# kv in 13 pieces by thirds of its rows, tile 0 scored third by third, and constant products between the pieces

## What is computed

```python
B, N, C = q.shape                      # 1, 12288, 128
kv_pool = kv.reshape(B, H // 4, 4, W // 4, 4, C).mean(axis=(2, 4))   # H = 384, W = 32
k = v = kv_pool.reshape(B, -1, C) @ w_sr                             # 768 keys
s = scale * (q @ k.transpose(0, 2, 1))
a = np.exp(s - s.max(-1, keepdims=True))
a /= a.sum(-1, keepdims=True) + 1e-09
x = a @ v
h = x @ w_in1;  x = (h / (1 + exp(-1.702 * h))) @ w_out1             # d_ff = 2048
h = x @ w_in2;  out = (h * clip(h + 3, 0, 6) / 6) @ w_out2
```

## Time and profile before

| | us |
|---|---|
| median of 3 runs (1280.7 to 1281.02) | 1280.78 |
| the profiled execution | 1280.32 |
| its span in the profile | 1278.6 |
| TensorE busy in the span | 1270.0 |
| VectorE, ScalarE busy | 1034.1, 1027.4 |

### The profile page before, as it was taken

The page is one execution under the profiler, slowest core; times in us unless marked ns, Lnnn a source line. Parts: engine busy times, 40 slices in busy tenths (PEclk is TensorE's granted clock), DMA queues, the critical chain, the costliest instruction groups (busy, mean ns, idle before and its releaser), DMA issues.

```text
span 1278.6 us, 18310 instructions
## 1 busy us (share of the span) xinstructions
PE 1270.0 (99%) x5800; PEld 1055.4 (83%) x5800; DVE 1034.1 (81%) x1084; ACT 1027.4 (80%) x1216; POOL 34.4 (3%) x46
## 2 busy tenths in 40 slices
PE   8999999999999999999999999999999999999998
PEld 7888888888888888888888888888888888888887
DVE  5788887888878878888788888887888878887768
ACT  3888877888788888887788878888888778887776
POOL 1800000000000000000000000000000000000000
PEclk9999999999999999999999999999999999999999
DMA  8421321303213123032130220311303213022001
GB/s 280 126 44 40 75 46 28 74 9 65 57 17 74 30 44 74 0 74 49 25 74 13 60 63 11 74 34 40 74 0 74 49 25 74 18 47 67 1 9 17
DMA packets 183685, 65.69 MB, mean 51 GB/s; under 512 B 104560, under 2 KB 176368, under 8 KB 183408
## 3 DMA queue, kind: packets, MB, share of 16 engines
q1 hardware_dynamic: 182576, 65.30, 22.3%
q10 hardware_dynamic: 1088, 0.13, 0.1%
HBM read 22.87 MB, written 6.34 MB: 23 GB/s over the span
## 4 chain that ended last, share of the span: by engine, by line
PE 97%; SPq 1%; DMA 1%; DVE 0%; ACT 0%; issue 0%; DVEq 0%
PE pair L1082 14%; PE pair L1083 14%; PE pair L1086 14%; PE bank_av L1082 9%; PE bank_av L1083 9%; PE bank_av L1086 9%; PE bank_out L1086 7%; PE bank_out L1083 7%; PE bank_out L1082 7%; PE score_banks L1086 2%; PE score_banks L1083 2%; PE score_banks L1082 2%; DMA kv_sb<-in_kv_dram 1%; SPq L354 0%; SPq L362 0%; SPq L366 0%
## 5 line engine op out<-in xcount | busy, mean ns | idle before, releaser
L912 DVE TENSOR_TENSOR mid_lo<-work,mid_hi 128x1024 fp32r<-128x1024 f32 (+1 forms) x193 | 233.9, 1212 | 112.5 <-ACT mid_hi L628 112.4
L1082 PE MATMUL pair<-x_hi,w_hi 128*128 128x512 f32 (+1 forms) x774 | 300.7, 388 | 0.0
L1083 PE MATMUL pair<-x_hi,w_lo 128*128 128x512 f32 (+1 forms) x774 | 300.0, 388 | 0.0
L1086 PE MATMUL pair<-x_lo,w_hi 128*128 128x512 f32 (+1 forms) x774 | 299.9, 387 | 0.0
L589 ACT ACTIVATE work<-pair 128x1024 f32<-128x1024 f32 x184 | 189.2, 1028 | 120.8 <-PE pair L1086 118.5
L904 DVE SCALAR_TENSOR_TENSOR work<-work,pair 128x1024 f32<-128x1024 f32 (+1 forms) x194 | 232.9, 1201 | 15.3 <-ACT work L616 14.6
L891 DVE TENSOR_TENSOR mid_lo<-work,mid_hi 128x1024 fp32r<-128x1024 f32 x184 | 223.6, 1215 | 25.1 <-ACT mid_hi L604 25.0
L616 ACT ACTIVATE work<-pair,half 128x1024 f32<-128x1024 f32 (+1 forms) x194 | 213.1, 1099 | 4.3 <-PE pair L1086 4.2
L628 ACT ACTIVATE mid_hi<-work 128x1024 fp32r<-128x1024 f32 (+1 forms) x193 | 201.8, 1046 | 2.3 <-DVE work L904 2.3
L604 ACT ACTIVATE mid_hi<-work 128x1024 fp32r<-128x1024 f32 x184 | 194.7, 1058 | 1.6
L1082 PEld LDWEIGHTS pair<-x_hi,w_hi 128*128 128x128 f32 x774 | 145.3, 188 | 33.7 <-ACT work L589 4.2
(11 more groups left out here) (175 smaller groups left out, 1560.2 us busy)
## 6 DMA issues: line engine op xcount, KB each, us to landing
p_keys<-p_turned SPq DMA_DIRECT2D x368, 96.0 KB, 2.2
inv_b<-inv_dram SPq DMA_DIRECT2D x23, 256.0 KB, 3.2
out_dram<-y_sb SPq DMA_DIRECT2D x92, 64.0 KB, 2.4
q_raw<-in_q_dram SPq DMA_DIRECT2D x88, 64.0 KB, 2.0
kv_sb<-in_kv_dram SPq DMA_DIRECT2D x6, 768.0 KB, 9.4
w_raw<-in_moe_w_in_dram SPq DMA_DIRECT2D x2, 1024.0 KB, 8.0
kv_sb<-in_kv_dram SPq DMA_DIRECT2D x6, 256.0 KB, 8.1
inv_dram<-inv_t SPq DMA_DIRECT2D x92, 0.5 KB
```

The lines of the kernel that those rows point to most:

```text
L912: dve.tensor_tensor(in_pair(mid_lo[mid2(t, p)], t, p, c), in_pair(act2[p % 2], t, p, c), in_pair(mid_hi[mid2(t, p)], t, p, c), ALU.subtrac ...
L1082: pe.matmul(dst, a_hi, b_hi, start=start, stop=False)
L1083: pe.matmul(dst, a_lo, b_hi, start=False, stop=False)
L1086: return pe.matmul(dst, a_hi, b_lo, start=False, stop=stop)
```

## The change

kv is loaded in 13 pieces by thirds of its rows: 128 image rows at a time, one row for each partition, two column groups (4 KB for each partition, 512 KB) in a piece, and the last two pieces one group (256 KB). Tile 0's q goes behind the fourth piece with a row of 2 KB for each partition, tile 1's q behind the last piece without a wait. A third of the rows gives a third of the keys (256), so the parts are now 256, 256, 128 and 128 keys, and a pooling product has 32 moving columns. VectorE adds four pixels to two for pieces 0 to 5 and to one for the others. One constant product of 288 columns stands between the early pieces.

Tile 0 is scored by thirds: all four slots against the first third of the keys between pieces 4 and 5, the second third around pieces 10 to 12, the last third behind the last piece. `early_maximum` takes the maximum of a slot over 512 keys, `late_maximum` that of two slots over the last 256, and a minimum (the values are negated) joins them for two slots at once. The high part of slot 0's turned probabilities is made by VectorE in place of ScalarE. GpSimd splits the inverse behind its first weight piece. PSUM banks are handed out anew. `PARTS` is 4, `SLOTS` 4 and `WIDE` 512. Cut to its core:

```diff
+        PART_AT = [0, CHUNK_KEYS, 2 * CHUNK_KEYS, 2 * CHUNK_KEYS + 128, KEYS]
+        PART_POOL = [bank_av[:, 0:CHUNK_KEYS], bank_av[:, 0:CHUNK_KEYS], bank_av[:, 0:128], bank_av[:, 128:256]]
+        PART_KEYS = [bank_out[:, 0:CHUNK_KEYS], bank_out[:, 0:CHUNK_KEYS], bank_out[:, 0:128], bank_out[:, 128:256]]
+        PARTS = 4
+
+        PIECES = [(a, g, 2) for a in range(CHUNKS) for g in range(0, KV_GROUPS, 2)][:-1] + [(2, 6, 1), (2, 7, 1)]
+        PART_PIECES = [4, 8, 10, 13]
+        SUMMED_FROM = 6
...
+        SECOND_BANK, FIFTH_BANK = pair[0][:, 512:1024], pair[1][:, 0:512]
+        VALUES_IN = [SECOND_BANK[:, 0:CHUNK_KEYS], FIFTH_BANK[:, 0:CHUNK_KEYS], SECOND_BANK[:, 0:128],
+                     bank_av[:, 256:384]]
...
+            def load_kv(a, first, groups, loaded):
+                src = kv_chunks[a][:, first * R * C:(first + groups) * R * C]
+                at = (a * KV_GROUPS + first) * R * C
+                sp.dma_start(kv_sb[:, at:at + groups * R * C], src).then_inc(loaded, 16)
+
+            for n, (a, first, groups) in enumerate(PIECES):
+                load_kv(a, first, groups, kv_loaded[n])
+                if n == 0:
+                    sp.dma_start(w_sr_sb[:, :], w_sr).then_inc(w_sr_loaded, 16)
+                if n == 3:
+                    sp.dma_start(q_raw[:, :], q_first).then_inc(q0_loaded, 16)
+            for n in range(4):
+                sp.dma_start(q_raw1[32 * n:32 * (n + 1), :], q_second[n]).then_inc(q1_loaded, 16)
...
-                if piece == 2:
+                if piece == 1:
...
+            q_high_first()
             pooled_copy(0)
             k_hi_copy(0)
-            q_high_first()
             v_hi_copy(0)
             pooled_copy(1)
+            k_hi_copy(1)
+            v_hi_copy(1)
             pooled_copy(2)
-            k_hi_copy(1)
             k_hi_copy(2)
-            v_hi_copy(1)
+            v_hi_copy(2)
+            pooled_copy(3)
+            k_hi_copy(3)
+            v_hi_copy(3)
             q1_copy()
             exponential(0, 0)
             exponential(0, 1)
-            p_hi_first(0)
             exponential(0, 2)
             p_hi_first(1)
             exponential(0, 3)
...
+            def add_pixels(n):
+                a, first, count = PIECES[n]
+                at = (a * KV_GROUPS + first) * R * C
+                groups = kv_sb[:, at:at + count * R * C].rearrange("p (g n) -> p g n", g=count)
+                dve.wait_ge(kv_loaded[n], 16)
+                half = dve.tensor_tensor(groups[:, :, 0:2 * C], groups[:, :, 0:2 * C], groups[:, :, 2 * C:4 * C],
+                                         ALU.add)
+                if n < SUMMED_FROM:
+                    half.then_inc(kv_added, 1)
+                    return
+                half.then_inc(kv_half_added, 1)
+                dve.wait_ge(kv_half_added, n - SUMMED_FROM + 1)
+                dve.tensor_tensor(groups[:, :, 0:C], groups[:, :, 0:C], groups[:, :, C:2 * C],
                                   ALU.add).then_inc(kv_added, 1)
 
...
+            def early_maximum(s):
+
+                if s < 2:
+                    dve.wait_ge(early_scored, 1)
+                else:
+                    dve.wait_ge(scores_ready, SLOTS)
+                at = first_scores_at(s, 0)
+                dve.reduce_max(early_max[:, s:s + 1], score_banks[:, at:at + WIDE], AX_X,
+                               negate=True).then_inc(max_part_ready, 1)
+
+            def late_maximum(m):
+                dve.wait_ge(scores_ready, 2 * m + 2)
+                at = first_scores_at(2 * m, CHUNKS - 1)
+                late = score_banks[:, at:at + 2 * CHUNK_KEYS].rearrange("p (s n) -> p s n", s=2)
+                dve.reduce_max(late_max[:, 2 * m:2 * m + 2], late, AX_X, negate=True).then_inc(max_part_ready, 1)
+                dve.wait_ge(max_part_ready, 3 * m + 3)
+                dve.tensor_tensor(neg_max[:, 2 * m:2 * m + 2], early_max[:, 2 * m:2 * m + 2],
+                                  late_max[:, 2 * m:2 * m + 2], ALU.min).then_inc(max_ready, 2)
+
+            def p_hi_first():
+                dve.wait_ge(pt_ready, 1)
+                dve.tensor_scalar(first_in_chunks(p_high, 0), turned_in(0), 1.0, None,
+                                  ALU.mult).then_inc(pt_hi_first_ready, 1)
...
+            for n in range(5):
+                add_pixels(n)
+            q_low_first()
             k_lo_part(0)
-            add_row_pixels(KV_GROUPS - 2, 0)
-            add_row_pixels(KV_GROUPS - 2, 1)
-            q_low_first()
-            add_row_pixels(KV_GROUPS - 2, 2)
-            add_row_pixels(KV_GROUPS - 1, 0)
-            add_row_pixels(KV_GROUPS - 1, 1)
-            add_row_pixels(KV_GROUPS - 1, 2)
+            add_pixels(5)
             v_lo_part(0)
+            for n in range(6, 10):
+                add_pixels(n)
             k_lo_part(1)
+            for n in range(10, 13):
+                add_pixels(n)
             k_lo_part(2)
-            maximum(0, 0)
+            v_lo_part(2)
             v_lo_part(1)
-            maximum(0, 1)
-            maximum(0, 2)
+            early_maximum(0)
+            k_lo_part(3)
+            early_maximum(1)
+            late_maximum(0)
+            v_lo_part(3)
+            early_maximum(2)
+            early_maximum(3)
+            late_maximum(1)
+            p_hi_first()
             p_lo_first(0)
-            maximum(0, 3)
             p_lo_first(1)
+            inverse_first()
...
+            def pool_piece(n):
+
+                a, first, count = PIECES[n]
+                part = [n < end for end in PART_PIECES].index(True)
+                if part > 0 and n == PART_PIECES[part - 1]:
+                    pe.wait_ge(pooled_ready, part)
+                pe.wait_ge(kv_added, n + 1)
+                pixels = 2 if n < SUMMED_FROM else 1
+                for g in range(first, first + count):
+                    at = (g - 4 if part == PARTS - 1 else g) * GROUP_KEYS
+                    for w in range(pixels):
+                        col = ((a * KV_GROUPS + g) * R + w) * C
+                        last = pe.matmul(PART_POOL[part][:, at:at + GROUP_KEYS], kv_sb[:, col:col + C],
+                                         patch[:, 0, :], start=w == 0, stop=w == pixels - 1)
+                if n + 1 in PART_PIECES:
...
+            def keep_busy(times, into=pair[2]):
 
                 for _ in range(times):
-                    pe.matmul(pair[2][:, 0:rows * GROUP_KEYS], ident[:, :],
-                              patch[:, 0:rows, :].rearrange("p a n -> p (a n)"), start=True, stop=True)
...
-            for g in range(1, 4):
-                pool_group(g)
-                keep_busy(3 if g < 3 else 1, rows=2)
+            keep_busy(3)
+            pool_piece(0)
+            keep_busy(1)
+            pool_piece(1)
+            keep_busy(1)
+            pool_piece(2)
+            keep_busy(1)
+            pool_piece(3)
+            turn_q_first(0)
             pe.wait_ge(w_sr_loaded, 16)
             keys_of(0)
-            pool_group(4)
             values_of(0)
-            turn_q_first(0)
-            pool_group(5)
-
-            pool_loaded_row(6, 0)
-            pool_loaded_row(6, 1)
+            keep_busy(1)
+            pool_piece(4)
             pe.wait_ge(k_lo_ready, 1)
             pe.wait_ge(q_lo_ready, 1)
-            scores_half(0, 0, 0)
-            pool_loaded_row(6, 2)
-            for a in range(KV_ROWS):
-                pool_loaded_row(7, a)
+            for s in range(SLOTS):
+                scores_first(s, 0)
+            pool_piece(5)
+            pool_piece(6)
+            pool_piece(7)
+            keep_busy(1, into=FIFTH_BANK)
             keys_of(1)
+            pool_piece(8)
+            values_of(1)
+            pool_piece(9)
+            pe.wait_ge(k_lo_ready, 2)
+            scores_first(0, 1)
+            scores_first(1, 1).then_inc(early_scored, 1)
             keys_of(2)
-            values_of(1)
-
+            values_of(2)
+            pool_piece(10)
+            pool_piece(11)
+            pool_piece(12)
+            scores_first(2, 1)
+            scores_first(3, 1)
+            keys_of(3)
+            values_of(3)
+            pe.wait_ge(v_lo_ready, 3)
+            turn_q_first(1)
             pe.wait_ge(k_hi_ready, PARTS)
-            scores_half(0, 0, 1, low=(k_lo_ready, PARTS)).then_inc(scores_ready, 1)
-            turn_q_first(1)
-            scores_half(0, 1, 0)
-            scores_half(0, 1, 1).then_inc(scores_ready, 1)
-            pe.wait_ge(v_lo_ready, 1)
-            scores_half(0, 2, 0)
+            scores_first(0, 2, low=(k_lo_ready, PARTS))
+            scores_first(1, 2).then_inc(scores_ready, 2)
             pe.wait_ge(q1_copied, 1)
-            scores_half(0, 2, 1).then_inc(scores_ready, 1)
+            scores_first(2, 2)
+            scores_first(3, 2).then_inc(scores_ready, 2)
+
+            pe.wait_ge(v_lo_ready, PARTS)
             turn_probs(0)
-            pe.wait_ge(v_lo_ready, 2)
-            scores(0, 3)
```

(14 more changed lines are left out.)

209 lines of the change are left out of this document (86 added, 123 removed).

## The result

| | before | after |
|---|---|---|
| median, us | 1281.02 (5 runs, 1280.7 to 1281.37) | 1289.86 (5 runs, 1287.33 to 1297.09) |
| ratio, 95% interval | | 1.0075 [1.0064, 1.0086] |
| span of the profiled execution | 1278.6 | 1288.1 |
| first product of the hidden layer (span's start = 0) | 42.08 | 51.07 |
| what follows it to the end of the span | 1236.5 | 1237.0 |

The change makes the kernel slower by 8.8 us, 0.7%. The profiled execution is the one at 1289.86; its mean granted clock is 0.993, that of the other four 0.998 to 1.000, and no profile shows where those lost their time. The forecast was 1280.1, the range ended at 1282.3, and slower had a chance of 0.08. Of the 9.5 us between the two spans 9.0 lie ahead of the hidden layer and 0.5 behind it.

What follows compares the result with a forecast made beforehand. The load bounds the first 22 us, TensorE with its chain the next 20; hidden layer 0.55 us sooner plus 0.1 from q's loading gives 0.65, so 1280.78 - 0.65 = 1280.1, range 1278.4 to 1282.3.

Steps and rivals of the forecast that it cites:

- rival 2: TensorE's clock falls; a spell inside the dense list costs 2.0 us, net 1.4 slower, 1282.2; chance 0.15, half past 0.2%.
- The load: Loading kv at the start: the landing curve is kept, last byte at 22.4 us, bounds 19.9 and 23.0.
- keys_of(0): First keys on TensorE, behind piece 3's pooling, q's turning and ScalarE's copies: start at 14.1 us.
- Pooling passes: TensorE's pooling matmuls of 32 columns while kv lands: 0.11 us each, bounds 0.09 and 0.125.
- rival 1: Exponentials don't hold TensorE and pieces land sooner, or faster passes and load: 1277.8 to 1278.2; chance 0.13.
- The dense list: TensorE's work from the first keys to tile 1's turned q, without room: 11.8 us, ending at 25.9.
- The strided reading of q: ScalarE and VectorE reading q's bank with a stride: between 0 and 0.6 us more, taken as 0.
- Idle 1.35: TensorE's wait for exponentials behind the last third's scores, before the first turned probabilities: 1.35 us.
- Scores of tile 1 to the hidden layer: TensorE's list from scores_second(0) at 31.05 to the hidden layer: 10.5 us, against 10.75 before.
- The minimum: VectorE's joining of two slots' early and late maxima ahead of the exponentials: 0.2 us.
- "All else keeps its order": Everything after 42.08, the hidden layer's start before, keeps its order apart from the names of banks.
- rival 3: The thirds of kv land out of step, piece 3 with piece 5, 2 us later: 1.35 us slower, 1282.1; chance 0.1.

Runs made afterwards that it cites:

- e5: The changed kernel with seven constant products in place of three ahead of piece 0; 1283.17 us, ratio 1.002.
- e9: e5 with the two maxima of a slot joined by a one-operand maximum in place of a two-operand minimum; 1282.14 us, ratio 1.001.
- e11: e10 with eight constant products ahead of piece 0 and none between pieces 0 to 3; 1280.81 us, ratio 1.0001.
- e10: e9 with ScalarE's copy of the first pooled part ahead of its copy of tile 0's q; 1281.50 us, ratio 1.0005.
- e7: e6 without the two constant products before piece 4 and before the keys of part 1; 1287.56 us, ratio 1.0043.
- e6: e5 with GpSimd splitting the inverse ahead of its first weight piece; 1282.49 us, ratio 1.0014.
- e13: The kernel before with its first four constant products of 288 columns cut into twelve of 96; 1281.03 us, ratio 1.0005.
- e4: The kernel before with one constant product behind each pooled group in place of four and three; 1281.18 us, ratio 1.0002.
- e2: The changed kernel with five, three and three constant products behind pieces 0, 1, 2 and three behind q's turning; 1286.97 us, ratio 1.0042.
- e8: e7 with VectorE adding four pixels to one for every piece; 1284.11 us, ratio 1.0024.

## Why the prediction was wrong

**The step that failed is rival 2's price and chance.** The mechanism and its signs were there ("matmuls of 288 columns at 0.5 us beyond 9 us"), and so was its rule, slower than by 0.2% when more than 6.5 us of dense work run at 1.2 GHz. But the length of a fall was taken from the cold start, 4.18 us, which gave 2.0 us and 1282.2. It lasted 17.1 us and cost 7.6 (e5 against after). Half of that, 3.80, was lost ahead of the dense list (first keys at 18.55 against 14.75), where the prediction had priced only a spell inside it. Nothing in the trace of before bounded the length of a fall, so the cost had no upper bound but the work itself (an estimate from the forecast's list: 11.8 us of dense work lose up to another 11.8), and the range had to reach toward it. The chance of 0.15 rested on 0.87 us of missing work in 10 to 20 us; the spell that decided lies at 7.7 to 9.5, behind piece 0, where the prediction noted one constant in place of four and let it stand at "two new idle spells of 0.6 to 1.1". It was 1.78. The Trainium skill ("TensorE: Matmul & The Clock Gate", HAM oscillation — how this bites in real kernels) was quoted for this rival. What it describes is a clock that falls again with each slice of data; the trace agrees that TensorE fell back when it waited for data, but shows one long fall behind one spell of 1.78 us. The outcome it stood for, slower, came; the pattern didn't.

The terms of the sum, read with the clock held (e5, e9 and e11):

- **The load** held. The changed kernel's rate was 414 to 424 GB/s from 12 to 18 us, above the 381 to 404 of before, but fell to 117 in the twenty-second us with only 0.34 of the transfer engines' time busy. The last piece was issued at 9.7 and landed 13.2 us later, at 22.9 (22.3 in e5), for a forecast of 22.4; SP, which waits for it, issues the first weights right behind (the issues of kv in ns, their time to landing in us, then the SP queue):

```profile
L377 SPq DMA_DIRECT2D kv_sb<-in_kv_dram x13: 400/477/1304, 0.8 to 9.7; - x13
...
DMA to landing us min/median/max: 4.3/9.8/13.2
...
22.91 0.34 SPq L398 DMA_DIRECT2D w_raw<-in_moe_w_in_dram  x1
```

  The 408.7 GB/s that the prediction cited from the Trainium skill ("DMA: Bandwidth & Descriptors", iDMA fabric — 4 AXI ports for 8 engines, asymmetric across TPBs) agrees with the middle of the load, but the end before 20 us that was estimated from it did not come. Nor did piece 3 land sooner than forecast (its adding starts at 11.23, at 10.97 in e5), so the gain of a faster load was not tested.
- **keys_of(0)** at 14.1: measured 14.75. Piece 3's adding ends near the forecast 11.6, but three constants and four pieces run back to back on TensorE from 8.12, so its pooling starts at 12.25: the front, not the landing, set the start. The wait for ScalarE's two copies, 1.05 us, was in the forecast (13.1 to 14.1), though not its remedy: e10 takes 0.46 away, and e11, without the constants between, 0.54 more.
- **Pooling passes** at 0.11: 0.10 to 0.11 (8 in the 0.81 us from 9.50 to 10.31 in e5, 32 in 3.49 in e11). The prediction priced a pass of 0.09 as 0.35 us in its band and as 0.9 in rival 1, and its three upper terms add to 1281.6, not 1281.4; neither decides anything. **The dense list** of 11.8 us: 11.96 (14.75 to 26.71). It is not TensorE's work alone: in e7, without its two constants, waits for other engines took most of their place. **The strided reading of q**: 0.60 and 0.69 us, nothing, as forecast. **Idle 1.35** ahead of the first turned probabilities: 1.28. **Scores of tile 1 to the hidden layer** 10.5: 10.35. These steps held.
- **The minimum** at 0.2: 0.16 and 1.09. The second put 0.9 us on the path, shown by e6 and e9 in two ways. It was priced by its size, without a look at what GpSimd runs at that time.
- **"All else keeps its order"** behind 42.08: order, yes, but not the moment at which an instruction load meets a transfer. 0.5 to 0.6 us, shown by e13.

From the forecast 41.55 to e5's 43.44: 0.65 for the later first keys, 0.16 for the list, 0.9 for the minimum, 0.3 between the list and tile 1's scores, less 0.15 behind them, in all 1.9. Then 0.6 at 74 and 7.6 for the clock. With the clock, the minimum and the front mended, e11 has its hidden layer at 41.57, where the forecast had it, and the time of the kernel before. It reaches 41.57 by other steps than the sum's (first keys 0.3 sooner), so that the two figures agree is in part luck.

**Rival 1** (more speed by a faster load) and **rival 3** (thirds late) didn't occur: the last piece landed no sooner than forecast, idle time stood before the first transposes, and piece 3's adding started at 11.23, forecast 10.9.

**Left open**: why the first rise of the clock comes at 6 in one execution and between 11 and 12 in another; what the four unprofiled executions of the changed kernel lost their time by; why an instruction load delays a landing by 1 us; and about 0.3 us by which the rest of e11's span is longer than that of before beyond the wait at 74 (its products lie 0.18 later at 77 us and 0.53 at the end, with no single wait between that shows it).

## What to carry to other kernels

When a change makes TensorE the limit where a load was, fill its idle spells before that point with constants, or gather the thin work into one unbroken run: a fall of the clock that was nearly free beside a load (0.2 us in e4) then costs half of the time that TensorE works under it (7.6 us here). Constants where there is no idle time cost by themselves (e2). Price a fall by the dense work that may lie under it, not by the last one you saw. A gain of half a us at the start is only had if the fixed things it moves against (GpSimd's list, code loading, weights) are looked up too.

## What the runs showed of the hardware

- An idle spell of 1.78 us ahead of thin passes (32 columns) brought 1.2 GHz for 17.1 us, though TensorE was over 90% busy in it. In e8 the clock fell among spells of 0.38 and 0.43 us, for 13.5 us. In e11 32 such passes in a row held it.
- A minimum of 128x2 values took 0.16 us alone and 1.09 beside a two-operand instruction of GpSimd; a subtraction over 128x1024 (both operands in SBUF) 1.22 and 2.04. A reduction at the same place took 0.16.
- A load of instructions (0.02 MB) at the moment of a transfer made its landing take 3.2 us in place of 2.2 (e13). Its place moved when TensorE instructions were added or taken away ahead of it (22.6, 18.7 and 20.7 us), but not in proportion to them.
